# Keep-busy matmuls behind the turn of k, u spread by TensorE, and a new order of the work around a decaying-state recurrence

## What is computed

```python
for t in range(S):                                   # S = 768
    cur = einsum('bhd,bhe->bhde', u[None] * kt, vt)
    y[:, :, t] = einsum('bhd,bhde->bhe', rt, state + cur)
    state = wt[:, :, :, None] * state + einsum('bhd,bhe->bhde', kt, vt)
x = y as [B, S, H*D]
h = gelu(x @ w_in);  u, v = halves of h              # x @ w_in: 384 -> 1024
v_s = w_sg @ (normalized v * g_ln) + b_sg            # over the 768 tokens
x = x + (u * v_s) @ w_out
u = x + (relu(x^T @ tok1) @ tok2)^T
out = u + relu(u @ ch1) @ ch2
```

## Time and profile before

| | |
|---|---|
| median of 3 runs | 416.8 us (415.47 to 416.86) |
| the profiled execution, its own time | 416.61 us |
| its span, first to last instruction | 415.1 us |
| PE, matmuls | 399.7 us busy (96%) |
| DVE | 176.7 us busy (43%) |
| ACT | 104.9 us busy (25%) |
| POOL | 178.9 us busy (43%) |
| loaded from and stored to memory | 28.12 MB read, 2.36 MB written |

### The profile page before, as it was taken

How to read it: one execution, slowest core, us unless ns; L and a number is a source line. 1 busy time by engine, 2 the same in 40 slices (tenths; PEclk the granted TensorE clock), 3 DMA queues, 4 the chain that set the end, 5 groups by cost and what they waited for, 6 DMA issues and landing times.

```text
span 415.1 us, 6126 instructions
## 1 busy us (share of the span) xinstructions
PE 399.7 (96%) x2354; PEld 371.4 (89%) x2354; DVE 176.7 (43%) x365; ACT 104.9 (25%) x192; POOL 178.9 (43%) x188
## 2 busy tenths in 40 slices
PE   6799999999987999999999999999999999999997
PEld 6688888888977999989999999888998899988996
DVE  6554457777872445230543575335002321123201
ACT  4033352565350102085200203124002310022100
POOL 5664449699993567089499993000000000000000
PEclk9555555899998999999999999999999999999999
DMA  7996735485611021100222330000010001000011
GB/s 204 253 257 183 216 104 148 125 218 172 198 38 39 1 77 31 47 0 12 67 51 64 117 112 4 0 0 2 19 39 19 2 0 39 19 19 2 0 39 38
DMA packets 16126, 30.88 MB, mean 74 GB/s; under 512 B 2016, under 2 KB 9696, under 8 KB 16096
## 3 DMA queue, kind: packets, MB, share of 16 engines
q1 hardware_dynamic: 16096, 30.48, 25.2%
HBM read 28.12 MB, written 2.36 MB: 73 GB/s over the span
## 4 chain that ended last, share of the span: by engine, by line
PE 95%; DMA 2%; issue 2%; SPq 1%; DVE 0%; DVEq 0%
PE bank L1101 25%; PE bank L1102 24%; PE bank L1103 24%; PE bank L1167 7%; PE bank L1120 4%; PE bank L1163 4%; PE bank L1203 2%; DMA vn<-in_v_rows 2%; PE bank L1144 2%; PE bank L1128 2%; PE bank L1139 1%; SPq L355 0%; SPq L349 0%; SPq L384 0%; SPq L360 0%
## 5 line engine op out<-in xcount | busy, mean ns | idle before, releaser
L782 ACT ACTIVATE ha_hi<-bank 128x512 fp32r<-128x512 f32 x36 | 21.5, 598 | 107.7 <-PE bank L1103 107.7
L1101 PE MATMUL bank<-c_hi,ha_lo 128*128 128x384 f32 x144 | 48.2, 335 | 0.0
L1103 PE MATMUL bank<-c_hi,ha_hi 128*128 128x384 f32 x144 | 48.1, 334 | 0.0
L1102 PE MATMUL bank<-c_lo,ha_hi 128*128 128x384 f32 x144 | 48.1, 334 | 0.0
L1011 DVE SCALAR_TENSOR_TENSOR ha_lo<-bank,ha_hi 128x512 fp32r<-128x512 f32 x36 | 24.9, 692 | 51.0 <-ACT ha_hi L782 51.0
L1103 PE MATMUL bank<-u2T_hi,c_hi 128*128 128x512 f32 x108 | 42.1, 390 | 0.0
L1102 PE MATMUL bank<-u2T_lo,c_hi 128*128 128x512 f32 x108 | 42.1, 390 | 0.0
L1101 PE MATMUL bank<-u2T_hi,c_lo 128*128 128x512 f32 x108 | 42.0, 389 | 0.0
L1167 PE MATMUL bank<-vn,am 128*128 128x48 f32 x192 | 36.5, 332 | 0.0
L1101 PE MATMUL bank<-sg_hi,z_lo 128*128 128x384 f32 x96 | 33.1, 344 | 3.3 <-issue 3.3
L1167 PEld LDWEIGHTS bank<-vn,am 128*128 128x128 f32 x192 | 35.4, 262 | 0.1
(11 more groups left out here) (135 smaller groups left out, 875.1 us busy)
## 6 DMA issues: line engine op xcount, KB each, us to landing
krT<-in_kr_turned SPq DMA_DIRECT2D x12, 448.0 KB, 4.3
kr<-in_kr_rows SPq DMA_DIRECT2D x12, 384.0 KB, 5.8
raw<-in_moe_w_ch SPq DMA_DIRECT2D x12, 384.0 KB, 3.1
vn<-in_v_rows SPq DMA_DIRECT2D x12, 192.0 KB, 5.5
raw<-in_moe_w_sg SPq DMA_DIRECT2D x6, 384.0 KB, 3.8
out<-x SPq DMA_DIRECT2D x11, 192.0 KB, 1.9
raw<-in_moe_w_in SPq DMA_DIRECT2D x4, 384.0 KB, 6.7
raw<-in_moe_w_tok SPq DMA_DIRECT2D x4, 384.0 KB, 3.2
```

The lines of the kernel that those rows point to most:

```text
L782: sc.activation(ha[0][:, i, :], bank[:, :], ACT.Relu).then_inc(act_out, 1)
L1101: te.matmul(dst, left[1], right[0], start=first, stop=False)
L1102: te.matmul(dst, left[0], right[1], start=False, stop=False)
L1103: return te.matmul(dst, left[0], right[0], start=False, stop=last)
```

## The change

- **Dummies.** The 12 identity matmuls at the start become 9, then the product that spreads u, then 4. In chunk 0 three more, and in chunks 1 to 4 two more, stand behind the turn of k.
- **The old state's sum.** The identity product of chunks 1 to 4 becomes `carry_state` and stands behind the turn, ahead of the dummies; it waits for `st` only, no longer for v and the copy of the turned k.
- **u.** One row of 384 numbers is loaded; PE multiplies ones with it (128x384), and ACT copies the bank to `ub`.
- **Loads.** u's row stands third; k's and r's rows of chunk 0 stand behind turned k of chunk 1 and v of chunk 0.
- **Diagonal and y.** `dg` has two buffers. POOL and DVE take `rku`, `diagonal` and `diagonal_v` in another order; `y_tile(n)` of DVE stands in chunk n + 1, behind `forward` and `diagonal` (behind the masks in chunk 5; chunk 0's behind `state(1)`); `count_range` stands behind the loop.
- **Splits.** ACT takes the high parts of `high` ahead of the slot-0 products from chunk 6 on (those of `w_out` excepted). POOL makes the last low part of `w_sg` ahead of the r, k, u products in chunk 10. Products in slots shift: `u` 5 from (9, 2) to (10, 0), `u` 7 to (10, 1), each `sg` one place later.

```diff
-    (9, 0): [("u", 0, 1)], (9, 1): [("u", 0, 3)], (9, 2): [("u", 0, 5)],
-    (10, 0): [("u", 0, 7)], (10, 1): [("sg", 0, 0)], (10, 2): [("sg", 0, 1)],
-    (11, 0): [("sg", 0, 2)], (11, 1): [("sg", 0, 3)],
+    (9, 0): [("u", 0, 1)], (9, 1): [("u", 0, 3)],
+    (10, 0): [("u", 0, 5)], (10, 1): [("u", 0, 7)], (10, 2): [("sg", 0, 0)],
+    (11, 0): [("sg", 0, 1)], (11, 1): [("sg", 0, 2)],
 }
-TAIL = ([("sg", 0, i) for i in range(4, 8)] + [("xT", 1, i) for i in range(6)] + [("out", 0, i) for i in range(6)]
+TAIL = ([("sg", 0, i) for i in range(3, 8)] + [("xT", 1, i) for i in range(6)] + [("out", 0, i) for i in range(6)]
...
+    u_row = at("u_row", Z + NC * FH - C, [1, C])
...
-                sp.dma_start(ub[:, :], u.rearrange("(a h) d -> a (h d)", a=1).to_broadcast([PART, C])).then_inc(ub_in, 16)
+                sp.dma_start(u_row[:, :], u.rearrange("(a h) d -> a (h d)", a=1)).then_inc(u_in, 16)
 
             load_w(0)
             load_krT(0)
+            load_u()
             load_w(1)
-            load_kr(0)
-            load_u()
             load_krT(1)
             load_v(0)
+            load_kr(0)
             load_w(2)
             load_kr(1)
             load_v(1)
...
-                    pool.wait_ge(ub_in, 16)
+                    pool.wait_ge(ub_in, 1)
...
-                                 dg[:, :].rearrange("p (h a) -> p h a", a=1).to_broadcast([PART, H, D]), ALU.mult
+                                 dg[:, n % 2, :].rearrange("p (h a) -> p h a", a=1).to_broadcast([PART, H, D]), ALU.mult
...
-                   9: [("w_sg", 4)], 10: [("w_sg", 5)]}
+                   9: [("w_sg", 4)]}
+            first = {10: [("w_sg", 5)]}
...
                 diagonal_v(n)
+                for piece in first.get(n, []):
+                    split_low(*piece)
...
             scale_k(0)
+            scale_k(1)
             rk_products(0)
+            scale_r(1)
             rku_products(0)
-            for n in range(2):
+            rk_products(1)
+            for n in range(1, YR):
                 scale_k(n + 1)
+                rku_products(n)
                 scale_r(n + 1)
+                if n == 1:
+                    diagonal_v(0)
                 diagonal_v(n)
                 rk_products(n + 1)
-                rku_products(n + 1)
-            for n in range(2, YR):
-                diagonal_v(n)
-                rk_products(n + 1)
-                scale_k(n + 1)
-                scale_r(n + 1)
-                rku_products(n + 1)
+            rku_products(YR)
...
-                    11: [("w_out", 0), ("w_out", 1)]}
+                    }
+            late = {NCH - 1: [("w_out", 0), ("w_out", 1)]}
             act.wait_ge(v_consts, V_CONSTS)
             sc.activation(junk[:, 0:1], w_low[:, :], ACT.Gelu_apprx_tanh).then_inc(table_in, 1)
             act.wait_ge(table_in, 1)
+            act.wait_ge(u_spread, 1)
+            sc.copy(ub[:, :], ps[7][:, 0:C]).then_inc(ub_in, 1)
...
+                if n > YR:
+                    for piece in high.get(n, ()):
+                        split_high(*piece)
...
-                if n:
-                    dve.wait_ge(base_done, n)
-                ve.tensor_reduce(dg[:, :], rku[:, n % 2].rearrange("p (h d) -> p h d", h=H), AX.X, ALU.add).then_inc(dg_done, 1)
+                if n > 1:
+                    dve.wait_ge(base_done, n - 1)
+                ve.tensor_reduce(dg[:, n % 2, :], rku[:, n % 2].rearrange("p (h d) -> p h d", h=H), AX.X, ALU.add).then_inc(dg_done, 1)
...
-                if n < 2:
+                if n == 1:
+                    diagonal(0)
+                if n:
                     diagonal(n)
-                if n:
-                    backward(n + 2)
-                if n == YR - 1:
-                    count_range()
+                if n > 1:
+                    y_tile(n - 1)
+                backward(n + 2)
                 state(n)
-                if n == 0:
-                    backward(2)
-                y_tile(n)
-                if n:
-                    diagonal(n + 1)
+                if n == 1:
+                    y_tile(0)
+            diagonal(YR)
+            count_range()
             bound_x()
             for n in range(YR, NCH):
                 mask(n, 0)
                 mask(n, 1)
+                if n == YR:
+                    y_tile(n - 1)
                 if n + 1 < NCH:
                     forward(n + 1)
...
+            def carry_state(n):
+
+                pe.wait_ge(st_done, states(n - 1))
+                te.matmul(b1[0:QP, 0:NP * D], ident[0:QP, 0:QP], st[0:QP, :, :].rearrange("c p d -> c (p d)"),
+                          start=True, stop=False)
+
             def state_products(n):
 
                 wait_ring(pe, v_in, n)
                 if n:
                     pe.wait_ge(st_done, states(n - 1))
                 carried = 0 < n < YR
-                if carried:
...
-            def keep_busy(m):
+            def keep_busy(m, bank=ps[7]):
 
                 for _ in range(m):
-                    te.matmul(ps[7][:, 0:PART], ident[:, :], ident[:, :], start=True, stop=True)
+                    te.matmul(bank[:, 0:PART], ident[:, :], ident[:, :], start=True, stop=True)
 
             pe.wait_ge(ident_made, 1)
-            keep_busy(12)
+            def spread_u():
+
+                pe.wait_ge(u_in, 16)
+                pe.wait_ge(v_consts, V_CONSTS)
+                te.matmul(ps[7][:, 0:C], ones[0:1, :], u_row[0:1, :], start=True, stop=True).then_inc(u_spread, 1)
+
+            keep_busy(9)
+            spread_u()
+            keep_busy(4, ps[6])
             for n in range(NCH):
                 scores(n)
                 if n % NC < NC - 1:
                     turn_kp(n)
+                if 0 < n < YR:
+                    carry_state(n)
+                if n < YR:
+                    keep_busy(2 if n else 3, ps[6] if n == 0 else ps[7])```

How the instructions stand, at three places. In the rows `kp` and `rp` are scaled k and r, `kn` the turned k, `st` the state, `am` the masked scores, `vn` v.

TensorE, from the start to chunk 1's dummies; before:

```order
L1257 MATMUL bank<-ident 128x128 x12
L1120 MATMUL bank<-rp,kp 128x128 x8
L1128 MATMUL bank<-ident,kp 128x112 x4
L1144 MATMUL bank<-vn,kn 64x48
...
L1167 MATMUL bank<-vn,am 128x48 x8
L1120 MATMUL bank<-rp,kp 128x128 x8
L1128 MATMUL bank<-ident,kp 128x112 x4
L1139 MATMUL bank<-st,ident 112x192
L1144 MATMUL bank<-vn,kn 64x48
```

More of the change, by code:

```diff
@@ L177, in build @@
     ones = put("ones", [PART, PART])
-    dg = put("dg", [PART, H])
+    dg = put("dg", [PART, 2, H])
     oki = put("oki", [PART, 1], I32)
@@ L226, in build @@
         ub_in, gln_in, bsg_in = sem("ub_in"), sem("gln_in"), sem("bsg_in")
-        ident_made = sem("ident_made")
+        ident_made, u_in, u_spread = sem("ident_made"), sem("u_in"), sem("u_spread")
         consts0, consts, v_consts, preset = sem("consts0"), sem("consts"), sem("v_consts"), sem("preset")
@@ L653, in chunk_end @@
                             if n == NCH - 1:
-                                split_low("w_out", i - 2)
+                                split_low("w_out", i - 1)
             def rest():
@@ L665, in rest @@
                     chunk_end(n)
-                for i in range(4, 8):
+                for i in range(3, 8):
                     split_gated(0, i)
@@ L837, in _ @@
                     normal(b, i)
-                for piece in high.get(n, ()):
+                for piece in (high if n <= YR else late).get(n, ()):
                     split_high(*piece)
@@ L1137, in state_products @@
                 carried = 0 < n < YR
-                if carried:
-                    te.matmul(b1[0:QP, 0:NP * D], ident[0:QP, 0:QP], st[0:QP, :, :].rearrange("c p d -> c (p d)"),
-                              start=True, stop=False)
                 for p in range(NP):
@@ L1264, in _ @@
                     turn_kp(n)
+                if 0 < n < YR:
+                    carry_state(n)
+                if n < YR:
+                    keep_busy(2 if n else 3, ps[6] if n == 0 else ps[7])
                 for job in slot_jobs(n, 0):
```

## The result

The changed kernel takes **390.86 us** (median of four runs, 390.61 to 391.33) against 416.81 (415.47 to 416.86, measured beside it): ratio 0.9386, 95% interval 0.9365 to 0.9407. The forecast was 392.0. The profiled run took 391.33, its span is 389.8 where before's is 415.1, and its mean granted clock 0.981 where before's is 0.918.

What follows compares the result with a forecast made beforehand. PE was taken to bound the kernel nearly throughout, at half clock for 65 us. From 416.6, minus 24.0 (up to chunk 7) and 3.1 (chunks 9 to 11), plus 1.3 for a dip and 1.2 for contention: 392 us, range 388 to 413.

Steps and rivals of the forecast that it cites:

- The start: Chunk 0: gap ahead of its scores closed, loads earlier; scores of chunk 1 at 13.9 instead of 17.11, 3.2 us.
- Chunks 1 to 4, clock held: PE at clock 1.00 takes 5.9 us a chunk instead of 10.97; scores of chunk 5 at 37.5 instead of 60.97.
- Chunk 5 at 1.00: about 8 us: Chunk 5 takes about 8 us instead of 14.0, held up by POOL's two low parts of `w_in`; chunk 6 at 45.5.
- What is late next: Chunk 6: PE waits 5.6 us for raw piece 4; chunk 7 starts at 61.3, 24.0 us gained, 1.3 possibly given back.
- Chunks 9 to 11: The 3.26 us wait for `w_sg` goes, the 0.94 at chunk 10 becomes 2.7; 3.1 us gained, one dip in all.
- The 1.2 us for contention: Whole kernel: 1.2 us added to the sum because three engines are now all at their limit.
- Rival 2: Clock lost in chunk 0 and not back before 70 us: 411.3, or 412.6 with a fall in chunk 10; chance 0.26.
- Rival 1: Clock lost once on the way or late, in chunks 1 to 4: 398 to 409 us; chance 0.16.
- Rivals 3 and 4: 3: clock lost early, slower by chunk 10's wait, 421.8 (chance 0.05); 4: order changes nothing at 0.50, 415 to 418 (0.04).

Runs made afterwards that it cites:

- Experiment 3: Changed kernel with the loads in the old order, u as 128 copies, no spread of u, 16 dummies at the start: 396.27 us, ratio 0.9509.
- experiment 1: Changed kernel without the 11 dummies behind the turn of k in chunks 0 to 4: median 405.26 us.
- experiment 2: Kernel before the change, plus only the dummies behind the turn and the state's sum ahead of them: 401.41 us, ratio 0.9677.
- experiment 6: Changed kernel with the range's flag made first, v of chunk 5 loaded earlier and 12 dummies in chunk 5: 390.78 us, ratio 0.9357.
- experiments 6 and 7: The second of these: the kernel of experiment 6 with ACT's high part of `w_in` 0 moved behind all of chunk 5: 391.7 us, ratio 0.9416.
- the first two of 5: Changed kernel with the range's flag made first: 391.21 us; the same with v of chunk 5 issued ahead of chunk 6's k and r: 389.96 us.
- experiment 8: Changed kernel with two identity transposes in place of each dummy behind the turn of k: 392.99 us, ratio 0.9407.

## Why the prediction was right, and where it was not

**The start: right.** Spread of u till 7.13 (7.0 forecast), scores at 8.22 undelayed, ACT's copy of `ub` 0.48 us (0.5), state products 10.68 (10.65), outputs till 13.23 (13.0), scores of chunk 1 at 13.89 (13.9). Bounding the small row's arrival by two near rows and taking the early end was good. Experiment 3 shows that the part as a whole is worth 5.4 us, more than the 3.2 of its step; in the profile it is 4.2, since a late v also costs the clock there.

**Chunks 1 to 4, clock held: right.** 5.87, 5.92, 5.92 and about 6.0 us where 5.9 was forecast; experiments 1 and 2 show the dummies to be the cause of the 1.00. The step also took the new order of DVE for a help; experiment 2 has chunks of 5.9 to 6.1 us without it. And the remark that up to 5 us of lateness in chunks 1 to 5 would cost nothing failed: in experiment 3 a start 4.3 us late is still 4.2 us at chunk 7.

**"Chunk 5 at 1.00: about 8 us" and "What is late next": wrong in mechanism, right in sum.** The step took chunk 5 as held up by POOL's low parts alone and put the lateness on raw piece 4 in chunk 6. What is late next is the flag, because DVE's `diagonal(5)` had been moved ahead of `count_range`: the diff showed this, and the prediction priced the order of `dg` and `rku` only by POOL's path from scores to scores. The wait of 3.2 us took the clock for ten microseconds of chunk 5, which took 14.8 us where 8 were forecast. Nor is the flag the whole of it: with flag and v out of the way and the clock at 1.00 throughout, chunk 5 still takes 11.3 us (experiment 6), and its chain there runs through DVE and POOL. Chunk 7 was forecast at 61.3, with 1.3 more if a dip falls there, and came at 62.71: 22.7 forecast and 22.6 measured, but the 5.6 us of idle time in chunk 6 are not there, nor the dip. Two errors of the same size stand in for each other, 6.8 us too few in chunk 5 and 6.8 too many in chunk 6 (17.1 forecast with the dip, 10.3 measured), and that is luck. Raw piece 4, forecast for 54.7, was there by 51.9 and 53.2 in experiments 6 and 7. It did not make PE wait in the kernel after because chunk 6 started 6.9 us later than forecast, and not in experiment 6 either, where it started at 48.76.

**Chunks 9 to 11: right in kind, its size in part open.** The wait of 3.26 us went and the one of 0.94 grew, to 1.62 where 2.7 was forecast, and the one dip of the sum is here. The profile gives 2.7 us, dip included, where the sum has 3.1 without a dip or 1.8 with it. Undoing this part costs 3.7 us between the two profiled executions: the waits are 2.6 of it (0.95 and 3.25 against 1.62), and the dip is longer. By the medians it costs 6.4, up to 3.1 of them from ACT's high parts ahead of the slot-0 products, which the prediction had priced for chunk 6 and at nothing here. What the other executions lost beyond the 3.7 us no profile shows.

**The 1.2 us for contention** were not needed: 390.8 without them, 390.86 measured. But that sum stands on the two errors above.

**Rival 2** (clock lost in chunk 0 and not back before 70 us, 0.26) rested on "nothing in 65 us brought it back". That held for the work that PE then had. With dummies between the narrow products it comes back within chunks 0 to 2, in the profiles of experiments 2, 3 and the first two of 5. Chunk 2 then starts 1.8 to 4.4 us later than in the kernel after, so a loss in chunk 0 would have cost 2 to 5 us, and the rival at 411 deserved less than 0.26; for the kernel without dummies it describes what experiment 1 measured (405). The range's upper end, 413, was wide for that reason. **Rival 1** is the nearest to what happened: one clock lost on the way, but behind chunk 4. **Rivals 3 and 4** did not come.

## What to carry to other kernels

Where TensorE is the bound and its granted clock reads one half, look at what it executes, not only at its busy share: a few full-width dummies at fixed places of each chunk were worth 14.4 us of 26 by the medians here, and they also bring a lost clock back. Once the clock holds, a remaining wait can cost twice, for itself and for the clock behind it, so try to fill the waits that you cannot take away. Here taking flag, v and the check's loads out of chunk 5 gave nothing certain in the time; with twelve dummies on top of the first two, the two executions of six whose clock held took about 4 us less than the kernel after, and with ten more at chunk 10 the clock held in all six and four of them took 387.4 to 387.9 us. When an order is changed on one engine, read every wait that now stands ahead of the signal that another engine needs; here one reduce ahead of the count put a wait of 3.2 us before PE, and the old order, with dummies, was as quick in the chunks that the new one was made for.

## What the runs showed of the hardware

- **A busy queue is not enough, and a lost clock can return.** 8.60 us of 8.60 busy with narrow products at 0.50 (before), 6.80 of 6.80 with dummies among them and then 1.00 (experiment 2); without the dummies PE stayed at 0.50 with 53.61 of 54.60 us busy, from 12.4 to 67 us (experiment 1). What of the dummies does it was not separated; transposes of the same width did as well (experiment 8).
- **Small differences in the mean clock go with about 4 us.** With chunk 5 filled, executions at a clock of 1.0 took 386.6 and 387.2, those at 0.990 to 0.995 took 390.6 to 392.6. That the fall alone makes this difference is not shown: two executions without the check's loads took 387.7 and 387.85 at 0.991, and two of the fastest kernel 390.1 and 390.5 at 1.0. Whether the clock falls differs between executions of one kernel: 393.67 against 405.1 to 405.8 in experiment 1.
- **The column of the granted clock can disagree with the durations.** In the profile of the fastest kernel the first scores took half-clock time, while the column reads 1.00 from 5 to 10 us:

```profile
5.00:10.00 5.00, 5.00 (x19) 3.47 (x20) 3.99 (x11) 2.27 (x4) 1.17 (x1) 1.00 1.04 311
```

```profile
9.60 2.00 PE bank L1136 x16
```

  (2.00 us, as in the earlier trace rows; 1.13 in the kernel after). That run took 390.07, and the median is 387.88. The first scores were as slow, 2.01 and 1.97 us, in the profiles of the flag first and of the kernel without the check's loads. What decides it at the start is open.
- **The 16 DMA engines moved 284 to 290 GB/s** for three slices on end in the kernel after, against 253 and 257 in two of the earlier trace rows. Over 5 us it is up to 347 (from 25 to 30 us), against 308 in the same stretch of the earlier trace rows.
